# A three-stage kernel on one core: the second operand of the block inverse is kept block-diagonal, its first update product is taken over all 128 partitions, and filling products follow the chain items of the last tile

## The reference

```python
k_n = k / (norm(k) + 1e-6)
for t in range(S):                      # S = 768, state is D x D for each head
    y[t] = q[t] @ state
    state = state + beta[t] * outer(k_n[t], v[t] - k_n[t] @ state)
x = y as rows                           # 3072 x 384
e = argmax(x @ w_gate); h = relu(x @ w1[e]); out = p[e] * sigmoid(x @ w_output_gate)[e] * (h @ w2[e])
result = maximum(out @ v1, out @ v2, out @ v3) @ v_out
```

## Time and profile before

| | |
|---|---|
| median of 3 runs | 1069.67 us (1061.57, 1069.67, 1069.88) |
| the profiled execution | 1061.8 us, span 1060.1 us |
| PE, DVE, ACT, POOL busy | 95%, 49%, 35%, 34% |
| granted TensorE clock, mean | 0.979 |
| attention, 0 to 451 us, granted clock by stretch | 20-60 us: 0.91; 60-100: 1.00; 100-140: 0.96; 140-220: 1.00; 220-260: 0.91; 260-420: 1.00; 420-440: 0.74; 440-460: 0.69 |
| experts and last layer | 1.00, but for 0.97 in 700-750 us |

### The profile page before, as it was taken

How to read it: one execution, slowest core, us unless ns; L and a number is a source line. 1 busy time by engine, 2 the same in 40 slices (tenths; PEclk the granted TensorE clock), 3 DMA queues, 4 the chain that set the end, 5 groups by cost and what they waited for, 6 DMA issues and landing times. The chain is left out here.

```text
span 1060.1 us, 28043 instructions
## 1 busy us (share of the span) xinstructions
PE 1008.5 (95%) x11748; PEld 883.5 (83%) x11748; DVE 522.3 (49%) x1109; ACT 375.6 (35%) x735; POOL 364.0 (34%) x275
## 2 busy tenths in 40 slices
PE   3899999999999999789999999998999999999998
PEld 3788888888888888669999999997788888888987
DVE  5567667775677765354444443442433333323332
ACT  3556566565566666122222222221312121212110
POOL 4545376554535342133564552634301010100000
PEclk9899999998999999689999999999999999999999
DMA  9222222221222120234542445322201010100000
GB/s 302 100 57 60 58 75 66 67 67 50 65 68 67 51 60 17 95 130 172 179 171 92 149 154 171 134 90 82 60 30 34 26 37 22 37 30 8 23 8 30
DMA packets 58044, 84.66 MB, mean 80 GB/s; under 512 B 28880, under 2 KB 52944, under 8 KB 55376
## 3 DMA queue, kind: packets, MB, share of 16 engines
q1 hardware_dynamic: 52272, 46.89, 14.3%
q0 software_dynamic: 5664, 36.18, 9.9%
HBM read 61.62 MB, written 21.43 MB: 78 GB/s over the span
## 5 line engine op out<-in xcount | busy, mean ns | idle before, releaser
L1159 PE MATMUL hb<-early,last_h 128*128 128x512 f32 x648 | 206.0, 399 | 0.5 <-DVE early L1303 0.5
L1159 PEld LDWEIGHTS hb<-early,last_h 128*128 128x128 f32 x648 | 120.4, 189 | 28.3 <-DVE early L1303 0.9
L1159 PE MATMUL hb<-early,last_l 128*128 128x512 f32 x324 | 128.4, 396 | 0.0
L750 POOL TENSOR_TENSOR n_base<-n_kb_a,cf 128x512 f16<-128x512 f32 x24 | 30.4, 1268 | 167.8 <-DVE n_kb_a L600 167.8
L610 DVE TENSOR_TENSOR p<-bank,cf 128x512 f16<-128x512 f32 x96 | 66.2, 690 | 36.0 <-PE bank L379 34.9
L552 ACT CAST t<-bank 128x512 f16<-128x512 f32 x96 | 56.5, 588 | 66.4 <-PE bank L372 66.1
L1196 POOL DMA_INDIRECT rows<-y_sorted,idx x24 | 24.5, 1022 | 155.1 <-PE ob L1227 151.8
L1159 PE MATMUL ob<-wo_h,early 128*128 128x384 f32 x288 | 75.1, 339 | 0.0
L1083 POOL TENSOR_TENSOR late<-w_raw,late 128x3072 fp32r<-128x3072 f32 x8 | 54.5, 6811 | 59.8 <-DVE late L1023 59.5
L1159 PEld LDWEIGHTS hb<-early,last_l 128*128 128x128 f32 x324 | 61.0, 188 | 14.8
L992 ACT CAST ht_h<-ht_bank 128x512 fp32r<-128x512 f32 x56 | 32.9, 587 | 109.4 <-PE ht_bank L943 55.4
(11 more groups left out here) (173 smaller groups left out, 2205.4 us busy)
## 6 DMA issues: line engine op xcount, KB each, us to landing
w_raw<-w POOLq DMA_DIRECT2D x14, 1536.0 KB, 7.7
kq_t<-qh SPq DMA_DIRECT2D x24, 256.0 KB
y_sorted<-y_sb SPq DMA_DIRECT2D x31, 192.0 KB, 1.9
x_in<-x_sorted SPq DMA_DIRECT2D x29, 192.0 KB, 2.5
k_raw<-kt_in SPq DMA_DIRECT2D x24, 192.0 KB, 2.4
v_in<-vh SPq DMA_DIRECT2D x24, 192.0 KB
k_own<-kh SPq DMA_DIRECT2D x24, 192.0 KB, 2.4
out<-o_sb SPq DMA_DIRECT2D x24, 192.0 KB, 1.8
```

Of the source, the lines that this page charges most:

```text
L1159: ins = pe.matmul(out, a[x], b[y], start=first and i == 0, stop=last and i == 2, skip_group_check=True)
```

## The change

`tt16` gets the form of `n_both`: `[P, U, 2, C]` with the zeros set by DVE at the start, and each ACT copy into it becomes two copies of 64 partitions. The first product of `update` becomes `both_heads`. The second product and the one of `inv` still take 64 x 64 quarters of `tt16`. For the last step of stream 1, three products of 128 x 512 (fp16, result not used) follow each of `ks`, `z`, `up` (both pieces), `yt` and `lg`: 8 items, 24 products.

```diff
-    tt16 = single("tt16", [P, U, C], F16)
+    tt16 = single("tt16", [P, U, 2, C], F16)
...
+    FILLED = ("ks", "z", "up", "yt", "lg")
...
-            nl, nb, t, tt, pr = (lambda s, u, x=x[st]: x[s, u, :] for x in (n_lo, n_base, t16, tt16, p16))
+            nl, nb, t, pr = (lambda s, u, x=x[st]: x[s, u, :] for x in (n_lo, n_base, t16, p16))
+
+            def tt(s, u):
+                return tt16[st][s, u, s.start // C, :]
...
-                each_head(tt, pr, tb).then_inc(upd_done[st], 1)
+                both_heads(tt16[st], lambda u: p16[st][:, u, :], tb).then_inc(upd_done[st], 1)
                 each_head(pr, tt, ttb).then_inc(upd_done[st], 1)
...
+        def chain_and_fill(k, par, st, what, e):
+            chain(k, par, st, what, e)
+            if k == STEPS - 1 and st == 1 and what in FILLED:
+                for _ in range(3):
+                    pe.matmul(bank[0][2][:, :], tri16, flat(t16[0]), start=True, stop=True, skip_group_check=True)
...
+        def to_diagonal(to, x):
+            for hh, s in enumerate(half):
+                ins = act.copy(to[s, :, hh, :], x[s])
+            return ins
...
             elif what == "turn":
-                act.copy(tt16[st][:], ttb).then_inc(tt_out[st], 1)
+                to_diagonal(tt16[st], ttb).then_inc(tt_out[st], 1)
...
                 act.copy(t16[st][:], tb).then_inc(t_out[st], 1)
                 act.wait_ge(upd_done[st], 2 * (LVS * k + lv - LV0) + 2)
-                act.copy(tt16[st][:], ttb).then_inc(tt_out[st], 1)
+                to_diagonal(tt16[st], ttb).then_inc(tt_out[st], 1)
...
+            dve.memset(tt16[st][:], 0.0)
```

More of the change, by code:

```diff
@@ L523, in _ @@
         pe.wait_ge(blank, 1)
-        run(lambda a, c, b, n: walk(a, c, b, n, inv, chain, lambda *x: None))
+        def chain_and_fill(k, par, st, what, e):
[3 more added lines that the diff above has]
+                    pe.matmul(bank[0][2][:, :], tri16, flat(t16[0]), start=True, stop=True, skip_group_check=True)
+        run(lambda a, c, b, n: walk(a, c, b, n, inv, chain_and_fill, lambda *x: None))
         pe.wait_ge(counted_ready, TILES + 1)
@@ L540, in inv @@
                 act.wait_ge(gram_out[st], 2 * k + 2)
-                for hh, s in enumerate(half):
-                    ins = act.copy(n_both[st][s, :, hh, :], n_kb_a[par][st][s, :, 0, :])
-                ins.then_inc(n_both_ready[st], 1)
+                to_diagonal(n_both[st], n_kb_a[par][st][:, :, 0, :]).then_inc(n_both_ready[st], 1)
             elif what == "high":
```

## The result

| | before | with the change |
|---|---|---|
| median | 1067.55 us (20 runs, 1054.11 to 1074.18) | 1077.24 us (20 runs, 1071.53 to 1090.59) |
| ratio to before, 95% interval | | 1.0122 (1.0088 to 1.0155), about 13 us slower |
| profiled execution | 1061.8 us, span 1060.1 | 1074.3 us, span 1072.6 |
| granted clock, mean | 0.979 | 0.982 |

By the medians of all 20 runs the difference is 9.7 us, 0.9%. A second set, on the same chip as the first experiments, gave 1.0135 (1.0079 to 1.0192).

The account below looks back on a forecast made before the run. PE's own list was taken as the bound between 60 and 420 us. Terms +6.2 + 0 + 0.5 - 1.7 = +5.0 gave 1066.8 us on the profiled execution, 1074.7 on the median's scale; it named 1071, range 1060 to 1081.

Parts of the forecast that it names:

- The switches: PE's updates: changing between quarter and whole products costs 0.09 us each, +6.2 us in all, between +3 and +8.
- 72 full drains: PE's updates: if each additional switch drained TensorE fully, 0.16 us each, 11.5 us instead of 6.5; not used in the sum.
- Nothing but PE's list is late there: Attention, 60 to 420 us: PE's own list is the bound, so all +6.2 us of the switches is on the path.
- rival 3: Attention: new switches and fewer products make PE's clock drop more, 19 us for 11 drops, 1086 to 1094 us; chance 0.12.
- more than one stretch either way: Sign against the prediction: the clock of 60 to 420 us changes by more than one stretch.
- ACT's copies at 0: Attention: 120 more copies give ACT 60 us more work but cost 0; without cover, 11 us.
- rival 4: Attention: `z`, `t` or `y_tile` arrive late behind a second half copy on ACT, +11 us, 1078 to 1086; chance 0.07.
- The blanks: Start: two more memsets on DVE delay the first reduction, +0.5 us, between 0 and +1.6.
- The tail: Last tile's chain: the fill recovers part of the half-clock loss, -1.7 us, between -3.5 and +1.5.
- The two collisions: Last tile: fill behind `z` of piece 0 and the following `up` delays queued products, +0.3 us each at full clock.
- The sum: Whole kernel: switches +6.2, copies 0, blanks +0.5, tail -1.7, together +5.0 us against the profiled execution.
- within 1%: Whole kernel: the measured time differs from before by no more than 1% (10.7 us); chance 0.78.

Follow-up runs that it names:

- the first experiments: Three parts of the change against the kernel before: no fill 1.0118, the fill alone 0.9994, block-diagonal `tt16` with copies and memsets only 1.0039.
- the six quarter executions: The kernel before, and it with the fill, a small q load, 64 or 96 products ahead, or fill plus 64 ahead; 11 periods take 371.9 us.
- the whole ones: The change twice, and it without fill, with a small q load, or with 64 or 32 products ahead; 11 periods take 381.3 us.
- the twelve executions: Six executions with quarter products and six with whole products; 11 periods take 371.9 and 381.3 us on average.
- e3: Kernel before plus block-diagonal `tt16`, its 120 copies and two memsets; both update products still on quarters, no fill: 1068.42 us, 1.0039 (0.9995 to 1.0083).
- e2: Kernel before plus only the 24 filling products: 1059.95 us, 0.9994 (0.9960 to 1.0027).
- e9: Kernel before with 64 products of 8 columns ahead of all others on PE: 1061.93 us, 0.9986 (0.9951 to 1.0021).
- e13: Kernel before with the 24 filling products and 64 products of 8 columns ahead: 1057.45 us, 0.9964 (0.9934 to 0.9994).
- e7: Changed kernel with 64 products of 8 columns ahead of all others on PE: 1067.78 us, 1.0043 of before (1.0012 to 1.0074).
- e10: Changed kernel with 32 products of 8 columns ahead of all others on PE: 1072.89 us, 1.0110 of before (1.0052 to 1.0169).

## Why the prediction was right and wrong

**The switches: the mechanism right, the size a little low.** Forecast +6.2 over 12 periods, 0.52 each; measured 0.63 each, 7.6, inside the range of 3 to 8. It is the largest term of the loss. The single distances are those of the earlier trace rows. What the sum lacked is 0.02 on each second product, 0.18 a period; it also took 0.02 too little for what the four updates behind `kt` and `yt` give back. The Trainium skill (TensorEngine Tiling (Array Packing), Key Properties) says that changing the tiling mode drains TensorE. The prediction's estimate for 72 full drains was 11.5, against 6.5 by the rows; measured are 36 x 0.18 = 6.6, so no full drain shows in these switches.

**"Nothing but PE's list is late there": wrong.** That was the sentence by which the list's sum was the forecast. PE stands still for some 14 us in the 11 periods, most of it at packet borders and at the one fixed place. That the total is the same in both kinds is luck. I read 38.46 busy of 40 us at 220 to 260 us as "1.5 us of idle time" and did not ask what it was; 1.23 of it was the instruction wait at 237 us, and 0.30 the fixed pause. Between the rows at 201.98 and 204.75 of the earlier trace rows lay another such wait, in rows that I left out there: `up`, one row of 8 products elsewhere, is cut in two with 0.74 us of "issue" between.

**The clock (rival 3): right in direction, wrong in cause.** It is worse kept in the periods: 23.6 us at half clock instead of 16.0 on average, +2.7 us, in the profiled pair +6.0. Of the 7.6 us more, 3.0 lie ahead of the first rise, which came at 27.6 to 33.9 us in the six quarter executions and at 28.3, 28.6 and 42.4 to 44.8 in the whole ones. The prediction's test was "more than one stretch either way", and five stretches instead of two failed it. The rival's cause, the short switches, is not what precedes the drops; long pauses are: of the 34 drops between 60 and 420 us in the twelve executions, 33 began during a pause over 0.65 us or within 3 us of its end. They followed 12 of the 32 waits of that length at packet borders with quarters and 21 of the 47 with whole products. Whether the smaller number of products, the rival's other half, makes a drop more likely after a pause is not shown. At 0.12 its chance was too low, for it adds to a list that was already at +5 and so needs little to pass 1%. Over 29 runs of the kernel before, the time rose by 0.41 us for each us at half clock (from their mean clocks), so the 0.5 that I took was near.

**ACT's copies at 0: right for the waits.** All that releases PE between 60 and 420 us with the change (line waited for, releaser, total, times, longest) is

```profile
PE bank L373 <- issue: 7.2, 7, 1.9
PE bank L391 <- issue: 1.2, 1, 1.2
PE chain L477 <- issue: 1.1, 1, 1.1
PE chain L514 <- issue: 0.9, 1, 0.9
```

No ACT among them, and rival 4 falls. Ahead of 60 us PE's waits for ACT's `t` are 2.3 us in all instead of 1.8. ACT at the two places of the earlier trace rows, with the change:

```profile
224.40 0.59 ACT L566 CAST t<-bank 128x512 f16<-128x512 f32 x1 [1.99 <-PE bank L380]
224.88 1.17 ACT L546 CAST tt<-bank 64x512 f16<-64x512 f32 x2
...
230.25 0.47 ACT L583 COPY y_tile<-chain 64x384 f32<-64x384 f32 x1
231.04 0.48 ACT L583 COPY y_tile<-chain 64x384 f32<-64x384 f32 x1 [0.32 <-PE chain L498]
```

The pair of copies takes 1.17, 0.58 more than one and not 0.5; over the kernel ACT is busy 69 us longer, where the prediction had 60. Before one `y_tile` no idle time is left, before the other 0.32. Still e3's interval leaves room for a few us that no wait shows.

**The blanks: right.** DVE at the start, and the first product of PE:

```profile
4.77 0.48 DVE L714 MEMSET tt<- 128x512 uint32 x1
...
6.10 0.95 DVE L671 TENSOR_REDUCE nrm<-ksq 128x16 f32<-128x768 f32 x1
```

```profile
9.94 1.09 PE L411 MATMUL bank<-cf,kn 128*128 128x128 f32 x4 [9.94 <-POOL kn L753]
```

The first product comes at 9.94 instead of 9.32, +0.62 for a forecast of +0.5, and the reduction no longer waits. The memset covers 1024 fp16 elements as 512 words in 0.48 us, which agrees with the Trainium skill (VectorE: DVE Perf Modes, Zero memsets can be issued as uint32). Whole and quarter kernels differ by +0.8 to the first `resid`, and the rest of the +2.8 in the profiled pair is the late rise of the clock: the change run again, with the rise at 28.3 instead of 43.2 us, has its first `resid` at 36.50 instead of 38.81.

**The tail: -1.7 expected, nothing measured.** In the profiled execution the clock was 1.00 from 415 to 463 us, and from `lg` of the other stream (426.65 before, 443.10 now) to the count it is 19.6 us instead of 24.1, more than forecast. But without the fill too the clock is often kept: time at half clock behind the last `resid` was 17.0, 3.8, 6.2, 10.0 and 13.9 us without and 0, 13.7, 10.2, 3.4 and 0 with it in the change. I had taken the one profiled execution, in which the kernel before lost 17 us of clock, for its usual one. The two collisions can cost up to 0.65 each, where 0.3 was taken. Together e2's -0.6 us, give or take 3.5.

**The sum.** +0.8 at the start instead of +0.5, +7.0 instead of +5.7 for the list of 11 periods, +2.7 instead of 0 for the clock and -0.3 for pauses, +0.7 instead of -1.2 from the last `resid` on: 10.8 instead of 5.0 (before rounding). The list was nearly right; the misses are the clock, at 0, and the tail, at -1.7. The range of 1060 to 1081 held because it was wide, built round two places of the runs, and not because the sum was right; the chance of "within 1%" at 0.78 was too high for a sum that stood at half of that bound with nothing in it for pauses and clock.

**What stays open.** Why the fixed pause of 0.5 us comes in some executions of the quarter kernels and not in others: e9 and e13 have the same list on PE until the last tile, and only e9 has it. Whether the time at half clock is longer because of the whole products: 16.0 against 23.6 us over six executions each, whose spreads (11.9 to 22.7, and 19.1 to 31.7) overlap. The same holds for the number of long waits, and for the late first rise of the clock. And what makes instruction packets late beside the q load. e7's advantage of 0.9% over the unshifted change is measured, but its pauses (12.0 us instead of 13.9 and 15.2) and its clock give no full account of it: e10 has nearly the same pauses (12.5) and is at 1.0110.

## What to carry to other kernels

When PE runs at its list, price a new form of product by the distance from block to block with its neighbours, not by the count of instructions: half as many products cost 7 us here, because each block of them stands beside blocks of another form. Lay one clean period of each kernel side by side, block by block; that is what tells a longer list from a pause. Before calling a period clean, look for a block that is cut in two with "issue" behind it, and compare minima over several executions and positions of the list. Take the tail's or the clock's state of one profiled execution as one draw, and check it against several before a term is built on it.

## What was not expected of the hardware

- PE waits for its own instructions: at borders of 256 instructions (16 KB) it stood 0.7 to 2.5 us, 4 to 9 times between 60 and 420 us, most of them at the same instruction when the program was run again. 128 more instructions ahead of everything moved the time of the change by 0.9% and of the kernel before by 0.1%; 64 and 192 more moved the change by 0.3% at most, inside its interval.
- Of 34 drops of the clock to 0.50 between 60 and 420 us, 33 began during such a pause or within 3 us of its end; 33 of 79 pauses were followed so, and others of like length (1.72 and 1.35 us in the change) were not.
- The record of the granted clock begins at its first rise, 27.6 to 44.8 us into the execution. PE was at half clock until then (a product of 64 columns took 0.24 us instead of 0.19), and the mean granted clock does not tell it.
- A quarter product's block cost 0.25 us and a whole one's 0.25 with its own kind behind it; each change of form added 0.08 to 0.10.
